# Limit search, limit closes and weight splits rearranged in an FFT and two-expert-layer kernel

## What is computed

```python
def _attn_ref(x):                       # x: 4 x 2496 x 256
    X = np.fft.fft(x, axis=1)
    X = np.fft.fft(X, axis=2)
    return X.real.astype(np.float32)

def _moe_ref(x, w_gate, w1, w2):        # N = 9984, D = 256, E = 8, F = 1024
    cap = N // E                        # 1248
    logits = x @ w_gate
    order = np.argsort(-logits.flatten())
    ...
    for idx in order:                   # largest logit first
        tok, e = (int(idx) // E, int(idx) % E)
        if assigned[tok] >= 0 or counts[e] >= cap:
            continue
        assigned[tok] = e
        counts[e] += 1
    ...
    out[mask] = np.maximum(x[mask] @ w1[e], 0.0) @ w2[e]

def _moe2_ref(x, w_gate, w_output_gate, w1, w2):
    e_idx = np.argmax(logits, axis=1)   # no cap here
    ...
    out[mask] = gate_w[mask, None] * eom[mask, e, None] * ye
```

## Time and profile before

| what | value |
|---|---|
| median of 3 runs | 1416.41 us (1414.52 to 1417.97) |
| the profiled execution's own time | 1416.52 us |
| its span, first to last instruction | 1414.8 us |
| PE busy | 1292.1 us (91%) |
| PEld busy | 1195.4 us (84%) |
| DVE busy | 764.1 us (54%) |
| POOL busy | 567.1 us (40%) |
| ACT busy | 325.4 us (23%) |
| mean granted TensorE clock | 0.921 |

### The profile page before, as it was taken

How to read it: one execution, slowest core, us unless ns; L and a number is a source line. 1 busy time by engine, 2 the same in 40 slices (tenths; PEclk the granted TensorE clock), 3 DMA queues, 4 the chain that set the end, 5 groups by cost and what they waited for, 6 DMA issues and landing times.

```text
span 1414.8 us, 31437 instructions
## 1 busy us (share of the span) xinstructions
PE 1292.1 (91%) x10842; PEld 1195.4 (84%) x10843; DVE 764.1 (54%) x1996; ACT 325.4 (23%) x788; POOL 567.1 (40%) x556
## 2 busy tenths in 40 slices
PE   5999788826999999998999996999999999999996
PEld 4657688825998998887999985999999999999996
DVE  2723788795768568875444454443333333333332
ACT  0103100012232323332333331212222222222221
POOL 2800042003647474745556553411344142444411
PEclk9999655557999999999999998899999999999998
DMA  9605442201122222221232212211223122232110
GB/s 350 222 1 187 164 150 64 89 1 34 64 65 64 72 71 65 71 64 64 72 100 78 76 56 77 91 49 45 68 73 103 42 74 71 76 101 73 45 41 20
DMA packets 70734, 116.25 MB, mean 82 GB/s; under 512 B 7784, under 2 KB 50545, under 8 KB 70640
## 3 DMA queue, kind: packets, MB, share of 16 engines
q1 hardware_dynamic: 46864, 72.36, 15.2%
q0 software_dynamic: 11808, 31.03, 6.8%
q10 hardware_dynamic: 11968, 11.63, 3.0%
HBM read 81.83 MB, written 34.45 MB: 82 GB/s over the span
## 4 chain that ended last, share of the span: by engine, by line
PE 73%; DVE 11%; issue 1%; POOL 1%; DMA 1%; ACT 1%; POOLq 0%; ACTq 0%; DVEq 0%
PE bank L1035 21%; PE bank L1037 21%; PE bank L1036 21%; PE bank L941 4%; PE bank L930 3%; DVE hot_r L1630 2%; PE bank L1174 1%; DVE arena L1533 1%; PE bank L1047 1%; DVE hot_q L1631 1%; DVE hot_q L1629 1%; POOL weights_low L667 1%; DVE hT_low L1783 0%; DVE xT_low L1776 0%; DVE arena L1577 0%
## 5 line engine op out<-in xcount | busy, mean ns | idle before, releaser
L1035 PE MATMUL bank<-weights_high,hT_high 128*128 (+1 forms) x1328 | 389.3, 293 | 3.3 <-DVE hT_low L2095 3.3
L1037 PE MATMUL bank<-weights_high,hT_low 128*128 (+1 forms) x1328 | 380.0, 286 | 0.0
L1036 PE MATMUL bank<-weights_low,hT_high 128*128 (+1 forms) x1328 | 378.9, 285 | 0.0
L1035 PE MATMUL bank<-xT_high,weights_high 128*128 128x256 f32 (+1 forms) x1072 | 337.5, 315 | 12.6 <-DVE xT_low L1776 8.7
L1037 PE MATMUL bank<-xT_high,weights_low 128*128 128x256 f32 (+1 forms) x1072 | 333.3, 311 | 0.0
L1036 PE MATMUL bank<-xT_low,weights_high 128*128 128x256 f32 (+1 forms) x1072 | 333.1, 311 | 0.0
L1035 PEld LDWEIGHTS bank<-weights_high,hT_high 128*128 128x128 f32 x1328 | 251.5, 189 | 3.6 <-issue 3.5
L1037 PEld LDWEIGHTS bank<-weights_high,hT_low 128*128 128x128 f32 x1328 | 251.6, 189 | 0.0
L1036 PEld LDWEIGHTS bank<-weights_low,hT_high 128*128 128x128 f32 x1328 | 251.2, 189 | 0.0
L1035 PEld LDWEIGHTS bank<-xT_high,weights_high 128*128 128x128 f32 x1072 | 205.5, 192 | 27.2 <-DVE xT_low L1776 9.8
L1037 PEld LDWEIGHTS bank<-xT_high,weights_low 128*128 128x128 f32 x1072 | 204.6, 191 | 11.7
(11 more groups left out here) (246 smaller groups left out, 1465.1 us busy)
## 6 DMA issues: line engine op xcount, KB each, us to landing
arena<-middle ACTq DMA_DIRECT2D x44, 258.0 KB
spectrum<-arena SPq DMA_DIRECT2D x39, 256.0 KB, 2.2
arena<-in_w2a_t SPq DMA_DIRECT2D x8, 1024.0 KB, 5.0
raw<-in_w1a SPq DMA_DIRECT2D x8, 1024.0 KB, 5.3
raw<-in_w2a SPq DMA_DIRECT2D x8, 1024.0 KB, 5.8
raw<-in_w1b SPq DMA_DIRECT2D x8, 1024.0 KB, 5.0
raw<-in_w2b SPq DMA_DIRECT2D x8, 1024.0 KB, 5.7
arena<-in_x SPq DMA_DIRECT2D x4, 768.0 KB, 4.6
```

The costliest lines, as they stand in the source:

```text
L1035: pe.matmul(out_, a[0], b[0], start=start, stop=False)
L1036: pe.matmul(out_, a[0], b[1], start=False, stop=False)
L1037: return pe.matmul(out_, a[1], b[0], start=False, stop=stop)
```

## The change

1. The bracket of the search is set from the logits of the first 23 of the 78 columns, in pieces (`bound`) on DVE between its feature copies 25, 31, 33 and 35, with the two PE steps between feature steps. Most memsets go along.
2. `step` no longer raises the floor in front of the next `compare`; `raise_floor` does so behind it. `name` leaves out the minimum for limit 0. `subtract` loses the surplus line; `shut` closes with a subtraction of 1e37 instead of a minimum, without the second `pen_e`; `left_open` moves to `reopen`, behind the next `compare`. In `rows` three linked operations replace five.
3. POOL's `add_given` and weight pieces wait for the last chunk of a compare.
4. `expert_of` of the fifth slot moves behind the one-hots, and in stage 1's closes behind `name`. `tokens(*LISTS[1])` moves from tile 42 to tile 44.
5. In stage 2 the second expert's 8 pieces are no longer split in front of the loop but asked for by `wants()`, like the others: at most 2 in each group until 8 are done.

```diff
+        BOUND_AT, BOUND_STEPS = 25, (29, 31, 33)
...
             pool.memset(given, 0.0).then_inc(s_given, 1)
-            add_given(0)
-            for c in range(SPLITS):
+            def behind_compare(ph, r):
+                pool.wait_ge(s_above, above_done(ph, r) + len(CHUNKS) - 1)
+
+            for ph in range(SERIAL):
+                if ph + 1 < SERIAL:
+                    behind_compare(ph + 1, 0)
+                add_given(ph)
+                for r in range(1, ROUNDS):
+                    c = (ph - 1) * (ROUNDS - 1) + r - 1
+                    if 0 <= c < SPLITS and ph + 1 < SERIAL:
+                        behind_compare(ph + 1, r)
+                        split(0, 0, c)
+            for c in range((SERIAL - 2) * (ROUNDS - 1), SPLITS):
                 split(0, 0, c)
-            for ph in range(1, SERIAL):
-                add_given(ph)
...
             pool.wait_ge(m2.want, 1)
-            for c in range(SPLITS):
-                split(E + 1, 1, c)
...
+            def bound(part):
+                if part == 0:
...
+                    dve.tensor_reduce(top[:], logits[:, 0:E * (BOUND_AT - 2)], AX.X, ALU.max,
+                                      apply_absolute_value=True).then_inc(s_bound, 1)
...
             for n in range(1, NB + 1, 2):
                 feature_out(dve, dve.tensor_copy, n)
+                if n == BOUND_AT:
+                    bound(0)
+                for part, at_ in enumerate(BOUND_STEPS):
+                    if n == at_ + 2:
+                        bound(part + 1)
...
                 link(dve.tensor_reduce(best[:, 0:NT1], src, AX.X, ALU.max))
-                link(dve.tensor_tensor(best[:, 0:NT1], best[:, 0:NT1], taken[:, 0:NT1], ALU.min))
+                if src is not log8:
+                    link(dve.tensor_tensor(best[:, 0:NT1], best[:, 0:NT1], taken[:, 0:NT1], ALU.min))
...
                 if r + 1 < ROUNDS:
-                    dve.tensor_scalar(probe[(r + 1) % 2], steps[:, (r + 1) * PROBES:(r + 2) * PROBES], move[:], low,
-                                      ALU.add, ALU.add)
+                    link(dve.tensor_scalar(probe[(r + 1) % 2], steps[:, (r + 1) * PROBES:(r + 2) * PROBES], move[:], low,
+                                           ALU.add, ALU.add))
+                else:
+                    raise_floor(link, r)
...
             def shut(link, src):
-                link(dve.tensor_scalar(pen_e[:], left[:], 0.0, FAR, ALU.is_le, ALU.mult))
-                link(dve.tensor_tensor(left_open[:], left[:], pen_e[:], ALU.add))
-                link(dve.tensor_scalar(pen_e[:], pen_e[:], -2.0, FAR, ALU.mult, ALU.add))
-                link(dve.tensor_tensor(open_log, src, each_j(pen_e), ALU.min))
+                link(dve.tensor_scalar(pen_e[:], left[:], 0.0, SHUT, ALU.is_le, ALU.mult))
+                link(dve.tensor_tensor(open_log, src, each_j(pen_e), ALU.subtract))
...
                         dve.sem_inc(m1.row, 1)
-                        tokens(link, *LISTS[1])
+                if n == PLACES_AT + 16:
+                    tokens(link, *LISTS[1])
...
-                link(dve.tensor_scalar(wf, wf, float((E + 1) * SPLITS), float((E + 2) * SPLITS), ALU.add, ALU.max))
-                dve.memset(want_i[:, 0:1], (E + 2) * SPLITS)
+                dve.memset(want_i[:, 0:1], (E + 1) * SPLITS)
...
```

More of the change, by code:

```diff
@@ L54 @@
 FAR = 1e38
+SHUT = 1e37
 HOTS = 6
@@ L903, in _ @@
                 pe.matmul(bk[0:m, 0:RC], s, feat_s[:], start=False, stop=True).then_inc(s_f_ps, 1)
+                if n == BOUND_STEPS[0]:
+                    pe.wait_ge(s_bound, 1)
+                    pe.transpose(bank[1][0:1, 0:P], top[:], cc("ident")).then_inc(s_bound_ps, 1)
+                if n == BOUND_STEPS[1] + 1:
+                    pe.wait_ge(s_bound, 2)
+                    pe.matmul(bank[1][:, 0:1], ones_f[:], top[0:1, :], start=True, stop=True).then_inc(s_bound_ps, 1)
             G = 6 if NT1 % 6 == 0 else 1
@@ L1474, in _ @@
                     feature_gates()
+            def bound(part):
+                if part == 0:
+                    for u in range(2):
+                        dve.wait_ge(s_out[u], BOUND_AT // 2 + u)
+                    dve.memset(ones_f[:], 1.0)
+                    dve.tensor_reduce(top[:], logits[:, 0:E * (BOUND_AT - 2)], AX.X, ALU.max,
+                                      apply_absolute_value=True).then_inc(s_bound, 1)
+                    dve.memset(zero_u[:], 0)
+                    dve.memset(ones8[:], 1.0)
+                    dve.memset(taken[:], FAR)
+                    dve.memset(gone[:], -FAR)
+                    dve.memset(left[:], float(CAP))
+                    link(dve.memset(left_open[:], float(CAP)))
+                if part == 1:
+                    dve.wait_ge(s_bound_ps, 1)
+                    dve.tensor_reduce(top[0:1, :], bank[1][0:1, 0:P], AX.X, ALU.max).then_inc(s_bound, 1)
+                if part == 2:
+                    dve.wait_ge(s_bound_ps, 2)
+                    link(dve.tensor_copy(floor[:], bank[1][:, 0:1]))
+                    link(dve.tensor_scalar(top_i[:], floor[:].bitcast(I32), 0x7F800000, None, ALU.bitwise_and))
+                    dve.tensor_scalar(width[:], top_i[:].bitcast(F32), 4.0, None, ALU.mult)
+                    link(dve.tensor_scalar(floor[:], top_i[:].bitcast(F32), -2.0, None, ALU.mult))
+                if part == 3:
+                    link(dve.tensor_scalar(steps, cc("parts"), width[:], None, ALU.mult))
+                    link(dve.tensor_scalar(probe0, steps[:, 0:PROBES], floor[:], None, ALU.add))
+                    for r in range(ROUNDS):
+                        ins = dve.tensor_scalar(step_b[:, r, :], ones_b[:], width[:], float(PROBES) ** -(r + 1),
+                                                ALU.mult, ALU.mult)
+                    link(ins)
             for n in range(1, NB + 1, 2):
                 feature_out(dve, dve.tensor_copy, n)
+                if n == BOUND_AT:
[3 more added lines that the diff above has]
+                        bound(part + 1)
             for u in range(2):
@@ L1670, in _ @@
                     if ph and r == 0:
-                        slots(link, ph - 1)
+                        reopen(link)
+                        slots(link)
+                        expert_of(link, ph - 1)
+                    if r:
+                        raise_floor(link, r - 1)
                     mark(ph, r)
@@ L1690, in _ @@
             shut(link, open_log)
+            reopen(link)
+            expert_of(link, SERIAL - 1)
             dve.wait_ge(s_hot_used, BATCHES)
@@ L1721, in routing @@
                         accept(link, ph)
+                if j == 0 and G in COMPARE_AT and COMPARE_AT[G][1]:
+                    raise_floor(link, COMPARE_AT[G][1] - 1)
                 if G in COMPARE_AT and COMPARE_AT[G][1]:
@@ L1731, in routing @@
                     counted_new(link, ph)
-                    subtract(link, ph)
-                    slots(link, ph)
+                    subtract(link)
+                    shut(link, open_log)
+                    reopen(link)
+                    name(link, open_log)
+                    slots(link)
+                    expert_of(link, ph)
                     if G == FINAL_AT:
                         expert_of(link, E - 1)
-                    shut(link, open_log)
-                    name(link, open_log)
                 if j == 3 and G in CLOSE_AT:
```

65 lines of the change are left out of this document (22 added, 43 removed).

## The result

The kernel after takes **1399.14 us** (median of 4 runs, 1398.48 to 1399.81), the kernel before 1416.51 (4 runs, 1414.52 to 1417.97): a ratio of 0.988, 95% interval 0.986 to 0.990. It is 17.4 us faster. The forecast was 1391.2 with a range of 1386.5 to 1400.0: the sign and the range hold, the range by 0.9, but 7.8 of the 25.2 us of the sum are missing. The profiled execution has a span of 1398.0, 16.8 less than before, so by the profile 8.4 are missing.

What follows compares the result with a forecast made beforehand. Bounds: a DVE-PE chain in the limit search; idle PE in the stages. Terms 3.4 + 9.0 - 2.4 + 0.6 + 0.2 + 2.4 + 0.2 + 6.8 + 5.0 = 25.2 us off 1416.4 gave 1391.2, range 1386.5 to 1400.

Steps and rivals of the forecast that it cites:

- rival (a): Search: POOL's new places cost 11.2 us instead of 2.4, giving 1400; chance 0.2.
- rival (b): Stage 1 gains stay away: idles at 434 and 650 stay over 2 us, about 1397; chance 0.13.
- signs of being wrong: Search shrinking by less than 5 us, token idle reappearing in the next group, or a stage 2 send late through pieces.
- The lower end of the range: 1386.5 us, reckoned with cost terms at their lower bounds, 3.6 + 0.7 less than the forecast.
- Bracket, 3.4: Start of the search: shorter bracket gains 4.1 us, less 0.7 at the transform's end, net 3.4.
- POOL out of limit 1, 9.0: Limit 1 of the search: moving POOL's splitting elsewhere recovers 9.0 us.
- POOL's new places, 2.4: Search: weight pieces behind compares cost 1.2 us and `add_given` at four closes 1.2, together 2.4.
- Floor sum, +0.6: Limit 4 of the search: floor sum behind the compare gains 0.19 us in three rounds, 0.6.
- PE holds that mark by the 6.99 of gate parts: Closes of limits 0 to 3: 6.99 us of gates cover the shorter close, otherwise worth 1.1 a limit.
- Closes in stage 1, 2.4 and 0.2: Fewer DVE operations before `x_out`: 2.4 us at 434, clock included, and 0.2 at the other close.
- Tokens 6.8: Stage 1, idle before 650: moving `tokens` gains 5.0 us plus 1.8 from the clock.
- second expert 5.0: Stage 2: splitting pieces by groups makes the first send earlier and recovers 5.0 us, clock included.

Runs made afterwards that it cites:

- e9: Kernel before with only the bracket set from the first 23 columns: 1414.05 us, ratio 0.9985.
- e1: Kernel after with POOL's work in the search put back in the order of the kernel before: 1402.18 us, ratio 0.991.
- e4: Kernel after with POOL's search work cut to the gap: ACT makes the casts, POOL subtracts, `add_given` goes in two halves: 1393.77 us, ratio 0.985.
- e6: Kernel after with the floor sum back in front of the next compare and the probe step unlinked: 1413.71 us, on the slower chip.
- e7: Kernel after with PE's gate parts spread otherwise: none behind the first move, 5 instead of 8 behind counts of limits 0 to 3: 1396.52 us, ratio 0.987.
- e5: Kernel after with `slots` and `expert_of` of a close in stage 1 moved behind the next `x_out`: 1396.31 us, ratio 0.986.
- e3: Kernel before with only the second expert's pieces asked for by `wants()`: 1408.23 us, ratio 0.9955.
- e8: Kernel after with e5, e7's gates, e4's POOL at one subtraction a limit, and small operations moved: 1383.47 us, ratio 0.977.
- e10: e8 with slot 0's raw weights loaded ahead of the fourth turned-weights load: 1397.50 us, ratio 0.976, on the slower chip.
- e11: Kernel after, unchanged, run again on the slower chip: 1410.63 us, kernel before there 1431.96, ratio 0.985.

## Why the prediction was right and where it was wrong

The sign and the large terms were right for the reasons given. That 1399.1 lies inside the range is less than that: the range went up to 1400 for rival (a), and what came is that rival's kind of cost at about half its size (6.1 of 11.2) with the first half of rival (b). One of the prediction's own signs of being wrong also came: from the first compare to the first operation of `rows` the search takes 163.0 (154.99 to 318.00) instead of 164.8 (158.24 to 323.05), which is 1.8 less and not at least 5. The lower end of the range was added up wrongly: with the costs at nothing 2.4 + 0.7 go, which gives 1388.1; the 3.6 used instead is found nowhere as a cost that was taken.

- **Bracket, 3.4.** The compare came 3.25 earlier, as said. The step that failed is the silent one: what starts earlier must find its data. The turned weights' loads are released by the last feature step, which the edit does not move, and 1.0 of it was lost again. Worth 2.3 in the kernel after; 1.8 in the profile of e9 and 1.9 in its median.
- **POOL out of limit 1, 9.0.** Right: in limit 1 the marks are 4.65 apart.
- **POOL's new places, 2.4.** This is the main error: about 6.1 (e1: the part nets 3.0). The overhang was reckoned against the next compare (2.0 against 1.69 + 0.19), but the first operation hit is the probe step, 1.3 after the compare's end, and it lasts until POOL is done. The prediction did name the probe step, and expected it at about 0.6, but gave the wait no price of its own. That gives 0.5 a piece, six times (0.1 was taken), and 1.4 in limit 4 (0.56 was taken). The `add_given` was right in kind (0.4 against 0.3, four times). The rule quoted in the prediction from the Trainium skill (SBUF — State Buffer, "SBUF: two separate sides"), an exclusive lock for the whole instruction, agrees with these rows: an operation of 0.17 to 0.30 that starts well inside a POOL instruction on SBUF ends with it, within 0.04 (0.85, 1.80), and one that starts 0.09 before its end (e4) keeps its size. It doesn't catch every operation: in the kernel before a DVE reduction (214.01, 0.80) and POOL's subtraction (214.52, 1.28) overlap, and neither is longer than alone. From these rows a piece is priced at POOL's end less where the probe step would have ended by itself, 217.84 - 217.33 = 0.5.
- **Floor sum, +0.6.** Worth next to nothing: the linked probe takes its full 0.30 and holds the compare for 0.33, and probe and floor sum together held it for 0.40. In e6 that is 0.4 over the whole search and 0.1 in limit 4.
- **"PE holds that mark by the 6.99 of gate parts".** True before; after, DVE holds it (e7), so the shorter close earned nothing there.
- **Closes in stage 1, 2.4 and 0.2.** Nothing came: the idle at the second one is 0.6 before and after. The row of 0.52 was read as the operation's own cost, but 0.35 of it was POOL's subtraction beside it, which ends at 427.92, 0.02 before the operation does. POOL in the kernel before:

```profile
426.63 1.29 POOL L667 TENSOR_TENSOR weights_low<-raw,weights_high 128x512 fp32r<-128x512 f32 x1
```

  With that operation gone, POOL's work hit the next ones: 0.87, 0.52 and 1.15 where 0.17 each is their size. Between count and `x_out` the small operations carry 1.7 of POOL's work before and 2.3 after. Count to `x_out` took 7.24 before and 7.17 after. Rival (b) named this outcome, at 434 though not at 650. Work moved behind `x_out` (e5) does what work removed in front did not.
- **Tokens 6.8, second expert 5.0.** Right: 6.7 and 5.0 in the profile. Two pieces, then a send, stand in the forecast order, the send at 892.9 rather than near 880; of the first two pieces the second is shown:

```profile
890.66 0.60 POOL L834 CAST weights_high<-raw  x1
891.43 1.30 POOL L836 TENSOR_TENSOR weights_low<-raw,weights_high  x1 [0.17 <-POOL weights_high L834]
892.88 1.01 POOL L822 DMA_INDIRECT out_y<-arena,tokb  x1 [0.15 <-issue]
```

Of the 8.4 missing in the profile 3.7 are thus POOL's places, 1.1 the bracket (1.0 of it the late weights), 0.6 the floor sum and 2.6 the closes, 8.0 together. The other 0.4 fits the clock's later rise at the start of stage 1 (5.7 instead of 4.9 behind the first hidden matmul, at half speed in between); no experiment separates that. The median has 7.8.

## What to carry to other kernels

Work put into a gap on a shared path is priced by when the *first* operation behind it wants to start, not by the gap's sum; cut it to fit (here ACT took the casts and an addition was halved) and it costs nothing at the marks here. A row's duration beside another engine's work holds that engine's share: take an operation's size from a row where it runs alone, for what is removed gives back only that. And where two engines hold a stage by turns, an edit on one can be worth nothing until the other is moved: fewer gate parts were worth 0 at a close alone, and about 1.7 with POOL fitted and the small operations out of the way.

## Unexpected of the hardware

- **The clock in stage 1 varies with little cause seen.** After the first hidden matmul it rises 3.1 to 6.1 later in thirteen profiles, 4.9 and 5.7 in two of the same kernel. The rise is read where the matmuls of 128x512 go from 0.63 to 0.40, in the kernel after at 334.3:

```profile
333.48 0.63 PE L1050 MATMUL bank<-xT_high,weights_low 128*128 128x512 f32 x1
333.91 0.60 PE L1048 MATMUL bank<-xT_high,weights_high 128*128 128x512 f32 x1
334.34 0.40 PE L1049 MATMUL bank<-xT_low,weights_high 128*128 128x512 f32 x1
```

  After an idle of 2.16 to 2.27 at the first close the clock falls at once or within 2 us, to 0.91 over 20 us, in six of ten profiles, and stays at 1.00 in three (e3, e4, e7). In the tenth (e6) it falls about 8 us later, behind a count in which PE stopped. With an idle of 0.77 it stayed at 1.00 in e5 and e8 and fell about 9 us later in e10. This moves a run by 2 to 3 us, so parts of this size were read from marks and idles, not from medians.
- **One chip was slower, and at one kind of place.** The chip of e6, e10 and e11 gave 1431.96 for the kernel before, against 1416. In e11 PE stops inside counts of 78 small matmuls in stage 1, waiting for nothing that the profile shows, and the clock falls behind it. PE's waits there (us in total, times, longest) and its window:

```profile
PE bank L955 <- issue: 6.4, 12, 1.1
```

```profile
400.00:420.00 20.00, 16.97 (x139) 0.83 0.10 34
```

The first profile of the kernel after has none of these stops. e6 and e10 have them too (6.2 in 13 and 6.9 in 11). The profile shows no cause for them, and none was tried.
